# A new beginning and another order of block stages in a four-engine pipeline of two gated layers

## The chip, the cores and the metric

The program runs on one core of a Trainium2 chip. TensorE (PE) multiplies matrices into PSUM; VectorE (DVE), ScalarE (ACT) and GpSimd (POOL) work element by element, POOL on SBUF alone; SyncE (SP) issues most transfers. The metric is the device time of one execution in microseconds.

## The reference

```python
def _attn_ref(x, weight):                 # x: (2, 4096, 192), weight: (8, 7)
    w = weight - np.max(weight, axis=-1, keepdims=True)
    w = np.exp(w)
    w = w / (np.sum(w, axis=-1, keepdims=True) + 1e-09)
    x_pad = np.concatenate([np.zeros((B, pad, D), dtype=np.float32), x], axis=1)
    idx = np.arange(S)[:, None] + np.arange(K)[None, :]
    x_unf = x_pad[:, idx, :].reshape(B, S, K, H, group)
    out = np.einsum('hk,bskhg->bshg', w, x_unf)

def _moe_ref(x, w_in, w_out):             # x: (8192, 192), w_in: (192, 2048)
    h = x @ w_in
    relu6 = np.clip(h + 3.0, 0.0, 6.0)
    g = h * relu6 / 6.0
    return (g @ w_out).astype(np.float32)

def _moe2_ref(x, w_in, w_out, a, b):
    h = x @ w_in
    h2 = h * h
    h3 = h2 * h
    P = a[0] + a[1] * h + a[2] * h2 + a[3] * h3
    Q = 1.0 + np.abs(b[0]) * np.abs(h) + np.abs(b[1]) * h2
    g = P / (Q + 1e-06)
    return (g @ w_out).astype(np.float32)
```

The first function's result goes through the second and then the third: a causal convolution of 7 taps with softmax weights per head, then two layers 192 to 2048 to 192 with different gates.

## The kernel before

Channels lie on partitions: 128 upper ones ("a") and 64 lower ones ("b"). The 8192 positions are 16 blocks of 512 columns, two batches taking turns (`k.off % 2`). The 2048 hidden channels are 16 tiles of 128 (`NF`), so a block is 16 tiles and the whole 256 (`NT`). Every fp32 operand of a matmul is split in a rounded part (`_hi`) and a rest (`_lo`); `in_product` has five matmuls of 128x512 for a tile (hi x hi, lo x hi, hi x lo for the upper channels, two for the lower ones, whose hi and lo share one operand `xb_hl`), and `out_product` five into two accumulators, `y0a_acc` and `y0b_acc` for layer 1, `y1a_acc` and `y1b_acc` for layer 2. With four banks for `h`, that is all of PSUM.

A tile of layer 1 goes: `in1` (PE), `relu1` (ACT), `gate1` (DVE, in place in `r1`), `g1hi` (ACT), `g1lo` (POOL), `out1` (PE). A tile of layer 2: `in2`; `lin2`, `abs2`, `sq2` (ACT); `num2`, `num1` (DVE); `den_sum` (POOL); `rsq2`, `rec2` (ACT); `newton`, `g_first`, `g_neg` (DVE); `g2hi` (ACT), `g2lo` (POOL), `out2`.

The order of each engine's work is written out by hand in `SCHEDULE`: for each engine a list of stages with a lag, and `emit` goes through it once per step p, issuing each stage for tile p - lag. Layer 2's tiles come 21 steps after layer 1's. Block stages (the convolution's taps, roundings of a block's input, moving an accumulator out) stand in the same lists, with the steps of a block at which they come, and a parity where every second block is meant. `conv_b` treats the lower channels of two blocks at once, its taps 1 to 3 (`conv_b_head`) in steps 11 to 13, 4 to 6 (`conv_b_tail`) in 26 to 28 of 32. 64 steps are unrolled, then a loop of 32 steps runs, then the rest is unrolled; behind tile 255 the lists are sorted by `LATE`.

Weights arrive in 16 chunks (8 for each layer, two tiles of `w_in` and `w_out` in each) through three staging tiles. Chunk c is split at `weight_step(c)`: POOL rounds `win_hi`, ACT rounds `wout`, DVE computes `win_lo` and both `wout` rests (`w_lo`), and `w_done` lets PE use the chunk. Chunk 0 is split by POOL and ACT ahead of the steps. The prelude loads the taps, normalises them on DVE and ACT, computes the first block's convolution with upper and lower taps taking turns, and a few scalars of layer 2 (`root`).

## Time and profile before

| | us |
|---|---|
| median of 3 runs | 1306.22 |
| lowest, highest | 1304.28, 1306.86 |
| the profiled execution | 1306.78 |
| its span, first to last instruction | 1305.0 |

A row of the timeline gives start, duration, engine, line of the kernel, operation, what it writes and reads, the shape and, in brackets, how long its engine was idle before it and what ended that. DVE and ACT instructions overlap their neighbours a little, so that the distance from start to start is about 0.1 us less than the duration. A busy engine is therefore judged by those distances.

### The profile page before, as it was taken

Reading aid. Unit: us, or ns where it says so; the run is one execution under the profiler, and the core shown is the slowest. Engines: PE = TensorE matmul, PEld = TensorE weight load, DVE = VectorE, ACT = ScalarE, POOL = GpSimd, SP = SyncE. Lnnn points to the kernel's source line nnn. Section 1 sums busy time; section 2 is a strip of 40 time slices with the busy share of each in tenths; the row PEclk is TensorE's granted clock in tenths of the full one; section 3 lists DMA queues with packets and bytes.
Section 4 is the critical chain, followed back from the end, with each engine's and each line's share of the span. In section 5 each row is a group of like instructions: output and inputs, shape, how many; then the busy total and the mean of one; then the engine's idle time right before and its main releaser. Section 6 shows DMA issues by size and latency. Waiting matters only on the chain.

```text
span 1305.0 us, 19385 instructions
## 1 busy us (share of the span) xinstructions
PE 1211.6 (93%) x5120; PEld 960.1 (74%) x5120; DVE 1209.7 (93%) x1806; ACT 1174.2 (90%) x2207; POOL 1052.3 (81%) x822
## 2 busy tenths in 40 slices
PE   3788999999999999999999999999999999999776
PEld 2666777777778777777777777787777877888654
DVE  6789999999999999999999989999999999998787
ACT  3459999999999999999999999999999999999896
POOL 2567888888888888887898888888888888988665
PEclk9989999999999999999999999999999999999888
DMA  3230000010000000000000100000000000000000
GB/s 103 71 101 5 5 21 1 1 30 1 21 1 21 10 1 20 1 20 10 21 0 1 29 1 21 1 14 16 1 20 1 20 1 6 8 1 13 1 13 12
DMA packets 10005, 21.00 MB, mean 16 GB/s; under 512 B 1712, under 2 KB 1712, under 8 KB 9904
## 3 DMA queue, kind: packets, MB, share of 16 engines
q1 hardware_dynamic: 9904, 20.01, 5.4%
q14 instruction: 81, 0.66, 0.2%
q8 instruction: 20, 0.33, 0.1%
HBM read 13.72 MB, written 6.29 MB: 15 GB/s over the span
## 4 chain that ended last, share of the span: by engine, by line
DVE 41%; issue 24%; ACT 22%; PE 10%; POOL 1%; ACTq 1%; DVEq 0%; DMA 0%; SPq 0%; POOLq 0%
DVE num L336 8%; DVE h L368 6%; DVE g L375 5%; PE h L231 5%; ACT g_hi L392 5%; DVE conv_a L479 4%; ACT num L319 4%; DVE num L341 4%; DVE r L302 4%; ACT h L358 3%; DVE conv_b L490 3%; ACT sqr L330 3%; DVE den L363 3%; ACT r L296 2%; ACT rsq L352 2%
## 5 line engine op out<-in xcount | busy, mean ns | idle before, releaser
L348 POOL TENSOR_TENSOR den<-den,sqr 128x512 f32<-128x512 f32 x256 | 338.6, 1323 | 188.5 <-ACT sqr L330 166.5
L312 POOL TENSOR_TENSOR g_lo<-r,g_hi 128x512 fp32r<-128x512 f32 x256 | 345.9, 1351 | 34.1 <-ACT g_hi L392 33.4
L386 POOL TENSOR_TENSOR g_lo<-g,g_hi 128x512 fp32r<-128x512 f32 x256 | 332.0, 1297 | 2.5 <-ACT g_hi L392 2.5
L302 DVE SCALAR_TENSOR_TENSOR r<-r,h 128x512 f32<-128x512 f32 x256 | 174.9, 683 | 36.7 <-ACT r L296 36.6
L341 DVE SCALAR_TENSOR_TENSOR num<-num,coef,h 128x512 f32<-128x512 f32 x256 | 191.2, 747 | 8.6
L392 ACT ACTIVATE g_hi<-r 128x512 fp32r<-128x512 f32 x256 | 166.6, 651 | 29.5 <-DVE r L302 23.8
L368 DVE SCALAR_TENSOR_TENSOR h<-num,coef,h 128x512 f32<-128x512 f32 x256 | 191.4, 748 | 0.0
L336 DVE TENSOR_TENSOR num<-num,h 128x512 f32<-128x512 f32 x256 | 174.6, 682 | 16.0 <-issue 6.0
L358 ACT ACTIVATE h<-rsq 128x512 f32<-128x512 f32 x256 | 155.1, 606 | 37.7 <-DVE num L341 37.0
L363 DVE SCALAR_TENSOR_TENSOR den<-den,h 128x512 f32<-128x512 f32 x256 | 174.0, 679 | 10.4 <-ACT h L358 8.3
L319 ACT ACTIVATE num<-h,coef 128x512 f32<-128x512 f32 x256 | 179.6, 702 | 0.0
L352 ACT ACTIVATE rsq<-den 128x512 f32<-128x512 f32 x256 | 163.8, 640 | 16.5 <-POOL den L348 13.2
L375 DVE SCALAR_TENSOR_TENSOR g<-den,h 128x512 f32<-128x512 f32 x256 | 174.1, 680 | 0.5
L392 ACT ACTIVATE g_hi<-g 128x512 fp32r<-128x512 f32 x256 | 166.1, 649 | 3.5 <-PE y1b_acc L249 2.3
L325 ACT ACTIVATE den<-h 128x512 f32<-128x512 f32 x256 | 154.1, 602 | 11.5 <-DVE g L375 8.8
L296 ACT ACTIVATE r<-h 128x512 f32<-128x512 f32 x256 | 153.5, 600 | 7.4 <-PE h L231 7.2
L330 ACT ACTIVATE sqr<-h 128x512 f32<-128x512 f32 x256 | 154.2, 602 | 3.4 <-PE h L231 3.4
L231 PE MATMUL h<-x0a_hi,win_hi 128*128 128x512 f32 x256 | 109.1, 426 | 48.8 <-POOL wout L402 21.3
L231 PE MATMUL h<-x1a_hi,win_hi 128*128 128x512 f32 x256 | 102.2, 399 | 18.3 <-DVE g L375 17.0
L231 PEld LDWEIGHTS h<-x0a_hi,win_hi 128*128 128x128 f32 x256 | 48.4, 189 | 89.3 <-DVE r L302 45.9
L243 PE MATMUL y0a_acc<-g_hi,wout 128*128 128x512 f32 x256 | 101.8, 398 | 10.8 <-ACT y_a L408 8.1
L243 PE MATMUL y1a_acc<-g_hi,wout 128*128 128x512 f32 x256 | 101.7, 397 | 5.6 <-POOL g_lo L386 3.4
(88 smaller groups left out, 2925.9 us busy)
## 6 DMA issues: line engine op xcount, KB each, us to landing
stage_w<-w_pack SPq DMA_DIRECT2D x16, 448.0 KB, 3.3
raw_a<-x_a SPq DMA_DIRECT2D x16, 259.0 KB, 3.6
out<-y_a SPq DMA_DIRECT2D x16, 256.0 KB, 2.6
raw_b<-x_b SPq DMA_DIRECT2D x16, 129.5 KB, 2.8
out<-y_b SPq DMA_DIRECT2D x16, 128.0 KB, 2.4
coef<-coefs SPq DMA_DIRECT2D x1, 3.0 KB, 1.6
tap_a<-taps SPq DMA_DIRECT2D x1, 3.5 KB, 1.6
tap_b<-taps SPq DMA_DIRECT2D x1, 3.5 KB, 1.9
```

The source lines that it names most:

```text
L231: mm = eng.matmul(psum, w, x[:, :], start=(i == 0), stop=(i == len(passes) - 1))
L302: eng.scalar_tensor_tensor(out=r[:, :], in0=r[:, :], scalar=1.0, in1=h1_of(q), op0=ALU.min, op1=ALU.mult).then_inc(S["gate1"], 1)
L312: eng.tensor_tensor(g1_lo[q.off % 2][:, :], r1[q.off % 2][:, :], f32(g1_hi[q.off % 2][:, :]), ALU.subtract).then_inc(S["g1lo"], 1)
L319: eng.activation(num[q.off % 2][:, :], h2_of(q), ACT.Identity, bias=a2, scale=reg_a3) \
L336: eng.tensor_tensor(n, n, h2_of(q), ALU.mult).then_inc(S["num2"], 1)
L341: eng.scalar_tensor_tensor(out=n, in0=n, scalar=a1, in1=h2_of(q), op0=ALU.add, op1=ALU.mult).then_inc(S["num1"], 1)
L348: eng.tensor_tensor(d, d, sqr[q.off % 2][:, :], ALU.add).then_inc(S["den_sum"], 1)
L363: eng.scalar_tensor_tensor(out=d, in0=d, scalar=Q_ONE, in1=h2_of(q), op0=ALU.add, op1=ALU.mult).then_inc(S["newton"], 1)
L368: eng.scalar_tensor_tensor(out=h2_of(q), in0=num[q.off % 2][:, :], scalar=a0, in1=h2_of(q), op0=ALU.add, op1=ALU.mult).then_inc(S["g_first ...
L375: eng.scalar_tensor_tensor(out=g2[q.off % 2][:, :], in0=den[q.off % 2][:, :], scalar=2.0, in1=h2_of(q), op0=ALU.subtract, op1=ALU.mult) \
L386: eng.tensor_tensor(g2_lo[q.off % 2][:, :], g2[q.off % 2][:, :], f32(g2_hi[q.off % 2][:, :]), ALU.subtract).then_inc(S["g2lo"], 1)
L392: return eng.activation(dst, src, ACT.Copy)
```

## The change

The prelude takes other ways. SP issues the upper taps and the upper channels first, then the lower ones, then the coefficients; chunk 0 is issued from ACT's queue. DVE normalises the upper taps and runs all seven upper taps, then `win_lo` of chunk 0 and `x0a_lo`, then the lower taps. PE begins with the three upper passes of tiles 0 to 3, and does the two lower ones for each of these tiles in its step.

In the first 22 tiles `gate1` writes its result into an accumulator of layer 2, which is not in use yet, and `g1lo` is computed by DVE. Weights are split by other engines: both roundings by ACT, all three differences by POOL, and chunks 1 to 15 are spread evenly over steps 0 to 20. `w_done` becomes two semaphores, one for each half of a chunk. In `SCHEDULE` block stages stand at other places of the same step, and `sq2` ahead of `abs2`.

```diff
@@ -21,23 +21,26 @@
+EARLY = 22
...
-    "scalar": [("cs_b_hi", AHEAD, 13, 0), ("x2a_hi", SUM1, 1), ("x2b_hi", SUM1, 0),
...
+    "scalar": [("x2b_hi", SUM1, 0), ("cs_b_hi", AHEAD, 13, 0), ("y2a_out", SUM2, 0),
...
-    "gpsimd": [("den_sum", 21), ("g1lo", 0), ("x2a_lo", SUM1, 0), ("g2lo", 23), ("cs_a_lo", AHEAD, 10)],
+    "gpsimd": [("den_sum", 21), ("cs_a_lo", AHEAD, 10), ("g1lo", 0), ("g2lo", 23), ("x2a_lo", SUM1, 0)],
...
         def pe_in1(eng, q):
-            first_block_weights(eng, 0, q)
+            split = ("cs_a_hi", "cs_a_lo", "cs_b_lo")
+            if q.loop is None and q.off < H_BANKS:
+
+                if q.off == 0:
+                    for tile in range(H_BANKS):
+                        first_block_weights(eng, 0, Step(tile), "w_in_done")
+                        in_product(eng, 0, Step(tile), h1_of(Step(tile)), split, range(3))
+                in_product(eng, 0, q, h1_of(q), split, range(3, 5)).then_inc(S["h1_done"], 1)
+                return
+            first_block_weights(eng, 0, q, "w_in_done")
...
         def pe_out2(eng, q):
+            first_block_weights(eng, 1, q, "w_out_done")
+            if q.loop is None and q.off == 0:
+                eng.wait_ge(S["g1lo"], EARLY)
...
+        def gated(q):
+
+            return [ya_acc[1], yb_acc[1]][q.off % 2] if is_early(q) else r1[q.off % 2]
...
         def relu1(eng, q):
             wait_count(eng, S["h1_done"], q, 1)
-            wait_count(eng, S["g1lo"], q, -1)
+            wait_count(eng, S["gate1" if is_early(q) else "g1lo"], q, -1)
...
         def gate1(eng, q):
             wait_count(eng, S["relu1"], q, 1)
-            r = r1[q.off % 2]
-            eng.scalar_tensor_tensor(out=r[:, :], in0=r[:, :], scalar=1.0, in1=h1_of(q),
-                                     op0=ALU.min, op1=ALU.mult).then_inc(S["gate1"], 1)
+            if is_early(q):
+                wait_count(eng, S["g1lo"], q, -1)
+            eng.scalar_tensor_tensor(out=gated(q)[:, :], in0=r1[q.off % 2][:, :], scalar=1.0,
+                                     in1=h1_of(q), op0=ALU.min, op1=ALU.mult).then_inc(S["gate1"], 1)
...
         def g1lo(eng, q):
+            if is_early(q) != (eng is nc.vector):
+                return
+            if not is_early(q):
+                wait_count(eng, S["g1lo"], q, 0)
             wait_count(eng, S["g1hi"], q, 1)
...
-        def w_lo(eng, c):
-            hi, lo, wo, raw_in, raw_out = w_views(c)
+            round_hi(eng, hi, raw_in).then_inc(S["wi_hi"], 1)
+            round_hi(eng, wo[:, :, 0:DA + DB], raw_out).then_inc(S["wo_hi"], 1)
+
+        def w_lo_in(eng, c):
...
         def weight_step(c):
 
 
-            return 2 * (c - 1) if c <= n_chunks else NF - 2 + c - n_chunks
+            return (c - 1) * (IN2 - 1) // (n_layers * n_chunks - 2)
...
-            run(eng, SCHEDULE["vector"], lambda c: w_lo(eng, c))
+            run(eng, SCHEDULE["vector"])
...
-            w_hi(eng, 0, "in")
-            w_lo(eng, 0)
-            w_hi(eng, 1, "in")
-            run(eng, SCHEDULE["gpsimd"], lambda c: w_hi(eng, c, "in"), early=1)
+            w_lo_out(eng, 0)
+            run(eng, SCHEDULE["gpsimd"], lambda c: (w_lo_in(eng, c), w_lo_out(eng, c)))
```

PE's first instructions, before and after; `x0a_hi` is the rounded upper input, `x0b_hl` the lower one. Before:

```order
L231 MATMUL h<-x0a_hi,win_hi 128x512
L231 MATMUL h<-x0a_hi,win_lo 128x512
L231 MATMUL h<-x0a_lo,win_hi 128x512
L231 MATMUL h<-x0b_hl,win_hi 128x512
L231 MATMUL h<-x0b_hl,win_lo 128x512
L231 MATMUL h<-x0a_hi,win_hi 128x512
```

After, the upper passes of tile 3 and what follows them:

```order
L236 MATMUL h<-x0a_hi,win_hi 128x512
L236 MATMUL h<-x0a_hi,win_lo 128x512
L236 MATMUL h<-x0a_lo,win_hi 128x512
L236 MATMUL h<-x0b_hl,win_hi 128x512
L236 MATMUL h<-x0b_hl,win_lo 128x512
L236 MATMUL h<-x0b_hl,win_hi 128x512
```

The lower passes of a tile no longer follow its upper ones: twelve upper passes stand ahead of the first lower one.

DVE in the first steps, behind the prelude: `r` is what `gate1` writes. Before:

```order
L302 SCALAR_TENSOR_TENSOR r_0<-r_0,h 128x512
L400 SCALAR_TENSOR_TENSOR win_lo<-stage_w,win_hi 128x512
L400 SCALAR_TENSOR_TENSOR wout<-stage_w,wout 128x2x128
L400 SCALAR_TENSOR_TENSOR wout<-stage_w,wout 128x2x64
L302 SCALAR_TENSOR_TENSOR r_1<-r_1,h 128x512
L479 SCALAR_TENSOR_TENSOR conv_a<-raw_a,tap_a,conv_a 128x512
```

After:

```order
L327 SCALAR_TENSOR_TENSOR y1a_acc<-r_0,h 128x512
L341 TENSOR_TENSOR g_lo<-y1a_acc,g_hi 128x512
L327 SCALAR_TENSOR_TENSOR y1b_acc<-r_1,h 128x512
L508 SCALAR_TENSOR_TENSOR conv_a<-raw_a,tap_a,conv_a 128x512
L341 TENSOR_TENSOR g_lo<-y1b_acc,g_hi 128x512
```

The three weight differences between two gates are gone from DVE, and a `g_lo` stands behind each gate.

DVE at a step with one of the lower taps 1 to 3, from `g_neg` on (`g`), then the gate (`r`), `newton` (`den`), `g_first` (`h`). Before:

```order
L375 SCALAR_TENSOR_TENSOR g_0<-den,h 128x512
L302 SCALAR_TENSOR_TENSOR r_1<-r_1,h 128x512
L363 SCALAR_TENSOR_TENSOR den<-den,h 128x512
L368 SCALAR_TENSOR_TENSOR h<-num,coef,h 128x512
L490 SCALAR_TENSOR_TENSOR conv_b<-raw_b,tap_b,conv_b 128x512
```

After:

```order
L404 SCALAR_TENSOR_TENSOR g_0<-den,h 128x512
L327 SCALAR_TENSOR_TENSOR r_1<-r_1,h 128x512
L392 SCALAR_TENSOR_TENSOR den<-den,h 128x512
L519 SCALAR_TENSOR_TENSOR conv_b<-raw_b,tap_b,conv_b 128x512
L397 SCALAR_TENSOR_TENSOR h<-num,coef,h 128x512
```

The tap has moved ahead of `g_first`.

## Rows read from the trace of the kernel before

**Rows 1.** The page, section 1: busy us, share of the span, instructions.
```profile
PE 1211.6 (93%) x5120; PEld 960.1 (74%) x5120; DVE 1209.7 (93%) x1806; ACT 1174.2 (90%) x2207; POOL 1052.3 (81%) x822
```

**Rows 2.** Timeline, steps 5 and 6: start, us, engine, line, operation, [idle before].
```profile
40.82 0.51 ACT L392 ACTIVATE wout<-stage_w 128x384 fp32r<-128x384 f32 x1
41.24 0.58 ACT L296 ACTIVATE r<-h 128x512 f32<-128x512 f32 x1
...
41.85 0.69 DVE L302 SCALAR_TENSOR_TENSOR r<-r,h 128x512 f32<-128x512 f32 x1 [0.94 <-ACT r L296]
...
42.57 0.64 ACT L392 ACTIVATE g_hi<-r 128x512 fp32r<-128x512 f32 x1 [0.75 <-DVE r L302]
42.81 0.39 PE L231 MATMUL h<-x0b_hl,win_hi 128*128 128x512 f32 x1
...
43.34 1.78 DVE L400 SCALAR_TENSOR_TENSOR win_lo<-stage_w,win_hi 128x512 fp32r<-128x512 f32 x1
...
44.17 0.39 PE L249 MATMUL y0b_acc<-g_lo,wout 128*128 128x512 f32 x1
...
45.71 0.50 PE L231 MATMUL h<-x0a_hi,win_hi 128*128 128x512 f32 x1 [1.16 <-DVE wout L400]
```

**Rows 3.** Timeline, the prelude and the first tile.
```profile
2.13 0.43 SPq L565 DMA_DIRECT2D raw_a<-x_a  x1
...
6.12 0.49 DVE L497 TENSOR_SCALAR conv_a<-raw_a,tap_a 128x512 f32<-128x512 f32 x1 [0.63 <-DMA raw_a<-x_a]
...
11.00 1.75 DVE L490 SCALAR_TENSOR_TENSOR conv_b<-raw_b,tap_b,conv_b 128x512 f32<-128x512 f32 x1
...
21.29 0.79 PE L231 MATMUL h<-x0a_hi,win_hi 128*128 128x512 f32 x1 [21.29 <-POOL wout L402]
...
23.82 0.60 ACT L296 ACTIVATE r<-h 128x512 f32<-128x512 f32 x1 [4.29 <-PE h L231]
```

**Rows 4.** Timeline, out1 of the second block, and relu1 of tile 21.
```profile
78.79 0.77 PE L243 MATMUL y0a_acc<-g_hi,wout 128*128 128x512 f32 x1 [3.15 <-ACT y_a L408]
...
91.41 0.60 ACT L296 ACTIVATE r<-h 128x512 f32<-128x512 f32 x1 [0.43 <-PE h L231]
```

**Rows 5.** Busy time by stretch: stretch, us, then each engine, PEclk, DMA, GB/s.
```profile
23.80:91.40 67.60, 53.46 (x201) 40.18 (x201) 54.04 (x76) 34.95 (x64) 38.32 (x36) 0.95 0.29 90
...
296.60:1138.00 841.40, 818.80 (x3517) 652.49 (x3516) 802.96 (x1197) 795.16 (x1502) 714.66 (x551) 1.00 0.04 10
```

**Rows 6.** Groups of DVE instructions, 120 to 1200 us: busy us, mean ns, idle before.
```profile
L341 DVE SCALAR_TENSOR_TENSOR num<-num,coef,h 128x512 f32<-128x512 f32 x227 | 169.5, 747 | 7.5
...
L302 DVE SCALAR_TENSOR_TENSOR r<-r,h 128x512 f32<-128x512 f32 x227 | 155.1, 683 | 21.0 <-ACT r L296 21.0
...
L479 DVE SCALAR_TENSOR_TENSOR conv_a<-raw_a,tap_a,conv_a 128x512 f32<-128x512 f32 x78 | 72.2, 926 | 0.0
L490 DVE SCALAR_TENSOR_TENSOR conv_b<-raw_b,tap_b,conv_b 128x512 f32<-128x512 f32 x38 | 45.6, 1200 | 0.0
```

**Rows 7.** Timeline of DVE and of POOL, a step with a lower tap.
```profile
667.99 0.68 DVE L302 SCALAR_TENSOR_TENSOR r<-r,h 128x512 f32<-128x512 f32 x1
...
669.85 1.41 DVE L490 SCALAR_TENSOR_TENSOR conv_b<-raw_b,tap_b,conv_b 128x512 f32<-128x512 f32 x1
...
669.40 1.30 POOL L348 TENSOR_TENSOR den<-den,sqr 128x512 f32<-128x512 f32 x1 [0.90 <-ACT sqr L330]
```

**Rows 8.** Timeline, DVE and ACT in steps 21 and 22.
```profile
96.10 1.71 DVE L400 SCALAR_TENSOR_TENSOR wout<-stage_w,wout 128x256 fp32r<-128x256 f32 x2
...
99.29 0.60 ACT L358 ACTIVATE h<-rsq 128x512 f32<-128x512 f32 x1 [2.12 <-DVE num L341]
```

**Rows 9.** Timeline of DVE, the gate of step 3 of an odd block.
```profile
620.39 0.69 DVE L302 SCALAR_TENSOR_TENSOR r<-r,h 128x512 f32<-128x512 f32 x1 [1.29 <-ACT r L296]
```

**Rows 10.** Timeline of ACT and of DVE, rec2 and the gate of a step with a tap.
```profile
629.09 0.60 ACT L358 ACTIVATE h<-rsq 128x512 f32<-128x512 f32 x1 [0.42 <-DVE num L341]
...
629.51 0.68 DVE L302 SCALAR_TENSOR_TENSOR r<-r,h 128x512 f32<-128x512 f32 x1
```

108 lines of the change are left out of this document (61 added, 47 removed).

## Prediction

> **What bounds the kernel now.** I read the page first, for the shares of the engines, then the busy time by stretch, then the timeline of the beginning, and last two blocks of the middle instruction by instruction. A "step" is one round of the order table; relu1 of its tile marks it, and a block is 16 steps. PE and DVE are both at 93%, ACT at 90% [rows 1]: no engine alone is the bound. PE's work can't be shortened: from 42.81 to 44.17 the trace has six matmul starts' distances, 0.227 us each [rows 2], and 5120 of them are 1161 us. The rest of the 1305 is lost at four places. Nothing runs on PE before 21.29 [rows 3]. Then relu1 of tile 0 starts at 23.82 and that of tile 21 at 91.41 [rows 3, 4]: 21 steps in 67.6 us, 3.2 each, although layer 1 alone asks PE for 10 matmuls, 2.27 us; only 201 matmuls start there [rows 5]. In the middle 11 blocks take 841.4 us [rows 5] where 3520 matmuls need 798: 43 us lost, 3.9 for each block of 76.5. The fourth is the drain of layer 2 behind the last tile, whose order this change leaves alone.
>
> **The change, part by part.** The sum is made against the profiled execution, 1306.8 us (span 1305.0 and 1.8 around it); it stands 0.6 above the median of the runs, 1306.2.
>
> *The time to the first gate.* Before, the first tap starts at 6.12, when raw_a is there, 3.99 after its issue at 2.13 [rows 3], and the seven taps of the upper channels alternate with seven of the lower. Now raw_a is issued second and not fourth, about 0.9 earlier, so it is there at 5.2. Seven taps alone are 0.49 + 6 x 0.75 [rows 3, 6], each behind the one before it; a handover from one instruction to the next takes 0.03 [rows 2]: 5.2 us. POOL takes differences of chunk 0 meanwhile; what that does shows at 11.00, a tap of 1.75 beside POOL's win_lo [rows 3]. I add one such collision, 1.0. conv_a is ready at 11.4, its rounding (0.63, as g1hi [rows 2]) at 12.1, and PE starts its upper passes there instead of at 21.29. That head start is worth little by itself, since no gate can run before the lower passes: cs_a_lo 0.7, the second taps' three small operations 0.6 (an estimate, below the 0.49 of a 512-column one each), conv_b 5.2 with 1.5 for POOL's chunk 1, its two halves 0.63 and 0.7: 21.4. Two lower matmuls, 0.79 at the most each and overlapped [rows 3], put relu1 of tile 0 at 22.5 instead of 23.82: **1.3 us**, between 3.8 with no collision and a loss of 1 with twice as many.
>
> *Steps 0 to 20.* What spoils them is DVE. The gate waits behind win_lo, which took 1.78 because POOL computed g1lo at that time, and behind two wout differences; PE then waited 1.16 for w_done [rows 2]. The change takes these three from DVE and gives them to POOL, which loses g1lo for 22 tiles; DVE gets that. It reads one operand from PSUM, as gate1 does, whose mean is 683 ns over 227 tiles with POOL busy beside it [rows 6]: so early g1lo costs DVE 0.7 and should not collide. 0.6 + 0.7 and at most one tap are 2.1 us in a step.
>
> What is late next is ACT. Its chain in a step: relu1 starts, 0.61 later the gate, 0.72 later g1hi [rows 2], and 0.52 later ACT is free (a rounding's 0.63 less the overlap): 1.85. win_hi and wout_hi of a chunk now both stand behind g1hi, 0.52 + 0.42 from start to start [rows 2]; a step with a chunk is 2.8, one without is PE's 2.27. Chunks 2 to 15 lie in steps 0 to 19 at even distances: 14 x 2.8 + 7 x 2.27 = 55.1. At step 18 out1 waits for y1a_out; before, that was 3.15 of PE [rows 4], ACT being late; I take 1.5, since ACT stays nearly as loaded. POOL needs 1.3 for win_lo [rows 7] and, by columns, 1.0 for wout: 2.3 for a chunk, less than 2.8. 1 us for the taps that meet it. Together 57.6 instead of 67.6: **10.0 us**. If ACT's chunks fell wholly in its idle time it were 50.6 (17 gained); if each of 14 chunks exposed another 0.5, 64.6 (3 gained).
>
> *The weights' transfers.* Chunk 3's load now stands behind the second raw_b, which waits for the last conv_b tap, at about 20. With raw_a's 3.99 it is there at 24; ACT wants it in step 1, about 26, PE in step 6. Hidden; if it took twice as long, ACT would wait 2 us once, and PE would not.
>
> *Steps 21 to 23.* DVE still has wout differences of 1.71 in front of num here, and ACT waits 2.12 for num1 [rows 8]. They are gone. I take **2.5 us**, between 1 and 3.5, the latter with the win_lo ahead of them.
>
> *The middle.* Per step, nothing is added or removed; block stages change place.
> - Lower taps 1 to 3 (conv_b_head) stood behind g_first, when POOL is in den_sum: one took 1.41 at 669.85, den_sum having started at 669.40 [rows 7]. Now they stand between newton and g_first, 1.2 behind the start of the gate. In that step the gate starts at 667.99, POOL falls idle at 668.50 and den_sum starts at 669.40 [rows 7]: the tap's new place, 669.19, lies in POOL's gap. It begins first, and POOL is pushed back by 0.5, of which it has 0.9. Three taps save some 1.9 us of DVE (3 x (1.41 - 0.75) and less), of which PE gets 1.0.
> - In step 3 of an odd block both x2a_hi and cs_b_hi stood ahead of relu1, and DVE idled 1.29 before the gate [rows 9]. cs_b_hi comes behind relu1 now: 0.2 to 0.5.
> - y2b_sum stands no longer ahead of num1, cs_a_lo no longer behind g2lo but ahead of g1lo, whose reader has two steps: 0 to 0.3 together, or a loss of 0.2.
> - The taps of conv_a move by 0.6 from one side of newton to the other, within the same gap: nothing.
> Sum 1.4 us for a pair of blocks, which loses 8. Seven pairs lie between tile 21 and the drain: **10 us**. The most would be all collisions of taps, whose means are 926 and 1200 ns against 747 for the same instruction on PSUM [rows 6]: 78 x 0.18 + 38 x 0.45 = 31 us. In an order laid around gaps of tenths a loss of 10 is the other bound.
>
> The Trainium skill ("SBUF — State Buffer", section "Who interferes with whom") says that a DVE instruction with two SBUF inputs and a GpSimd instruction that reads SBUF exclude each other for the length of an instruction, and whichever starts first goes first; one with at most one SBUF input does not contend. The trace agrees: 1.75 and 1.41 for taps, 683 ns for the gate. By that rule the new beginning has a danger of its own, and it is rival 4.
>
> **Sum.** 1.3 + 10.0 + 2.5 + 10 = 23.8; 1306.8 - 23.8 = 1283.0 for a profiled execution, 1282.4 on the median's footing.
>
> **The rivals.**
> 1. *Only the beginning gains.* For it: in the middle DVE is busy 803 and ACT 795 of 841 us [rows 5], so a gap closed at one place opens at the next. Against it: what a collision adds is work on DVE, not waiting, and it vanishes. Time 1306.2 - 13.8 = 1292.
> 2. *The middle gains more*, since taps of conv_a fall in POOL's gap too where they now don't: 20 to 30 there, 1262 to 1272.
> 3. *Slower: newton loses its cover.* Before, a tap of conv_a between gate1 and newton gave ACT 0.66 more to finish rec2. At 629.09 rec2 starts, released by num1, and ends at 629.69; the gate at 629.51 ends about 630.11 [rows 10]: 0.42 to spare without the tap. ACT now does cs_b_hi and conv_b_first ahead of rec2, and a den_sum pushed back makes rsq2 later. What rec2 then comes late by more than 0.42 is lost in each of the nine tap steps of a block, 126 in all. At 0.11 us each the beginning's 13.8 is eaten; at 0.25 it is 31 us, 1323. Against it: rec2 waited for num1, not for rsq2 [rows 10].
> 4. *POOL's 42 weight differences hold the taps.* Each can hold a tap of the early steps for its 1.3 us. There are 12 such taps; all held cost 15.6 instead of my 1, the beginning gives nothing, the middle as forecast: 1296. For it: POOL works 32 us of 55 there. Against it: in most steps DVE waits for ACT anyway, 0.7 us.
>
> **How the numbers follow.** Forecast 0.45; rival 1 0.18; rival 2 0.17; rival 3 0.10, most of it over 1309; rival 4 0.10. The range holds the forecast, rivals 1 and 4 and the nearer part of rival 2: 1267 to 1297. A measurement of this kernel can tell 0.2%, 2.6 us, from no change: faster than 1303.6 0.88, within 0.04, slower 0.08.
>
> **What would show it.** First matmul near 12, relu1 of tile 0 near 22.5 and of tile 21 near 80, with ACT rather than DVE filled in the chunk steps. In the middle a block near 75.8, mean of the lower taps under 1000 ns, and POOL's den_sum lengthened in their place. Wrong would be: relu1 of tile 21 later than 86, the taps as long as before, or idle time before newton that rec2 ends.

## The result and the profile after

The changed kernel takes 1261.53 us (median; 1260.44 to 1261.88), the kernel before 1306.39 (1304.28 to 1306.86) beside it. The ratio is 0.9653, with a 95% interval of 0.964 to 0.9665: 45 us faster, where 24 were forecast, and 5.5 us below the lower end of the range, 1267. In the profiled executions the span went from 1305.0 to 1258.6 us, 46.4 less.

The page of the changed kernel, section 1, answers to [rows 1]:

```profile
PE 1197.9 (95%) x5120; PEld 964.5 (77%) x5120; DVE 1170.4 (93%) x1784; ACT 1170.5 (93%) x2223; POOL 1080.1 (86%) x828
```

DVE is busy for 39 us less and POOL for 28 us more. Of the work itself DVE gave up the weight differences and took 22 early `g1lo`; the rest is taps that became shorter and, on POOL, `den_sum` that became longer.

The starts of `relu1` in the two traces share out the 46.4 us (tile 0 and 21 of before in [rows 3, 4], tile 240 as the end of a stretch in [rows 5]):

| stretch | before, us | after, us | gain | forecast |
|---|---|---|---|---|
| to tile 0 | 23.8 | 22.7 | 1.1 | 1.3 |
| tiles 0 to 21 | 67.6 | 57.8 | 9.8 | 10.0 |
| tiles 21 to 24 | 15.6 | 13.9 | 1.7 | 2.5 |
| tiles 24 to 32 | 37.2 | 35.7 | 1.5 | |
| tiles 32 to 240 | 993.8 | 962.8 | 31.0 | 10 |
| from tile 240 | 166.9 | 165.6 | 1.3 | |

The beginning, which is the first three rows, came out near what was worked out, 12.6 us against 13.8. The forecast's 10 us for the middle are those of seven pairs of blocks, most of them in the stretch from tile 32 to 240. Nearly all of the error is there.

**The beginning.** The timeline of the changed kernel, prelude and first tile (start, us, engine, line, operation, idle before):

```profile
6.10 0.48 DVE L526 TENSOR_SCALAR conv_a<-raw_a,tap_a 128x512 f32<-128x512 f32 x1
6.61 5.10 DVE L508 SCALAR_TENSOR_TENSOR conv_a<-raw_a,tap_a,conv_a 128x512 f32<-128x512 f32 x6
...
12.52 0.77 PE L236 MATMUL h<-x0a_hi,win_hi 128*128 128x512 f32 x1 [12.52 <-ACT x0a_hi L421]
...
21.45 0.80 PE L236 MATMUL h<-x0b_hl,win_hi 128*128 128x512 f32 x1 [4.05 <-DVE x0b_hl L429]
...
22.71 0.60 ACT L320 ACTIVATE r<-h 128x512 f32<-128x512 f32 x1 [2.03 <-PE h L236]
```

This answers to [rows 3]. PE begins 8.8 us earlier, then stands again until the lower channels are rounded, and the first `relu1` comes 1.1 us earlier. The six upper taps take 0.85 each. The first of the seven still starts at 6.10, as before (6.12), although its channels were asked for 0.9 us earlier: they landed 4.6 us after the issue at 1.20, and DVE's list has an operation on the lower taps ahead of it, which waits for their transfer until 6.02.

Two steps of the early stretch, answering to [rows 2]:

```profile
40.72 1.30 POOL L431 TENSOR_TENSOR win_lo<-stage_w,win_hi 128x512 fp32r<-128x512 f32 x1 [2.11 <-ACT win_hi L421]
40.96 0.59 ACT L320 ACTIVATE r<-h 128x512 f32<-128x512 f32 x1
41.58 0.70 DVE L327 SCALAR_TENSOR_TENSOR y1b_acc<-r,h 128x512 f32<-128x512 f32 x1 [0.72 <-ACT r L320]
41.98 1.61 POOL L431 TENSOR_TENSOR wout<-stage_w,wout 128x256 fp32r<-128x256 f32 x2
42.18 1.08 DVE L508 SCALAR_TENSOR_TENSOR conv_a<-raw_a,tap_a,conv_a 128x512 f32<-128x512 f32 x1
```

The gate writes into an accumulator (`y1b_acc`), DVE waits for ACT before it, and the tap that meets POOL's differences takes 1.08 instead of 0.75. The 8 upper taps of that stretch have a mean of 1068 ns: 2.6 us of collisions in all, on an engine that waits for ACT anyway.

`out1` of the second block waited 3.15 [rows 4] and still waits, now 3.43; `relu1` of tile 21 is 10.9 earlier:

```profile
70.70 0.47 PE L248 MATMUL y0a_acc<-g_hi,wout 128*128 128x512 f32 x1 [3.43 <-ACT y_a L437]
...
80.53 0.60 ACT L320 ACTIVATE r<-h 128x512 f32<-128x512 f32 x1 [0.90 <-PE h L236]
```

**The middle.** Busy time by stretch (as [rows 5]; the second stretch is again 11 blocks):

```profile
22.70:80.50 57.80, 51.05 (x192) 37.78 (x192) 39.98 (x56) 40.68 (x78) 40.24 (x44) 0.91 0.35 113
277.20:1093.00 815.80, 807.87 (x3519) 656.38 (x3518) 784.89 (x1198) 786.99 (x1502) 739.52 (x551) 1.00 0.04 11
```

3520 matmuls at 0.227 us need 798 us, so 17.8 us are lost in 11 blocks where 43 were lost before. DVE has 18 us less to do for the same instructions, POOL 25 more. The groups of DVE, 120 to 1160 us, show whose they are:

```profile
L370 DVE SCALAR_TENSOR_TENSOR num<-num,coef,h 128x512 f32<-128x512 f32 x225 | 168.3, 748 | 8.0
...
L508 DVE SCALAR_TENSOR_TENSOR conv_a<-raw_a,tap_a,conv_a 128x512 f32<-128x512 f32 x78 | 58.3, 747 | 0.0
L519 DVE SCALAR_TENSOR_TENSOR conv_b<-raw_b,tap_b,conv_b 128x512 f32<-128x512 f32 x36 | 32.3, 898 | 0.0
```

Against [rows 6] the upper taps fell from 926 to 747 ns, which is what `num1` takes with an operand in PSUM, and the lower ones from 1200 to 898. The mean of 926 hides that only 31 of the 78 upper taps were long: all 26 of steps 1 and 4, at 1.23 to 1.28 us, and 5 of step 8 at 0.96. All 31 had started while POOL was in `g2lo`. The one of step 4, tile 68, before and then after:

```profile
317.29 1.31 POOL L386 TENSOR_TENSOR g_lo<-g,g_hi 128x512 fp32r<-128x512 f32 x1
317.91 1.25 DVE L479 SCALAR_TENSOR_TENSOR conv_a<-raw_a,tap_a,conv_a 128x512 f32<-128x512 f32 x1
```

```profile
298.52 0.75 DVE L508 SCALAR_TENSOR_TENSOR conv_a<-raw_a,tap_a,conv_a 128x512 f32<-128x512 f32 x1
298.86 1.57 POOL L377 TENSOR_TENSOR den<-den,sqr 128x512 f32<-128x512 f32 x1 [0.32 <-ACT den L354]
```

What was taken from the taps shows on POOL, whose `den_sum` is the page's first group, of before and then of after:

```profile
L348 POOL TENSOR_TENSOR den<-den,sqr 128x512 f32<-128x512 f32 x256 | 338.6, 1323 | 188.5 <-ACT sqr L330 166.5 <-ACT den L325 22.0
```

```profile
L377 POOL TENSOR_TENSOR den<-den,sqr 128x512 f32<-128x512 f32 x256 | 376.9, 1472 | 130.0 <-ACT den L354 129.1
```

And one place answers to [rows 7], a lower tap in its new place behind newton, with POOL beside it:

```profile
633.15 0.75 DVE L519 SCALAR_TENSOR_TENSOR conv_b<-raw_b,tap_b,conv_b 128x512 f32<-128x512 f32 x1
633.29 1.77 POOL L377 TENSOR_TENSOR den<-den,sqr 128x512 f32<-128x512 f32 x1 [0.22 <-ACT den L354]
```

The tap starts 0.14 ahead of `den_sum` and runs at its full speed; `den_sum` takes 1.77 instead of 1.30. Before, the tap started second and paid 1.41. POOL has idle time for it (130 us are left before `den_sum`), but it isn't free: ACT's `rsq2` waits 20.3 us for `den_sum` between 120 and 1160 us, where it waited 10.8.

Which waits this ended is in the views of waits (total, times, longest). ACT and DVE of the kernel before:

```profile
ACT h L358 <- DVE num L341: 37.0, 92, 2.1
```

```profile
DVE r L302 <- ACT r L296: 36.6, 50, 3.5
```

The same two of the changed kernel, and a third of its DVE:

```profile
ACT h L387 <- DVE num L370: 6.9, 21, 1.6
```

```profile
DVE den L392 <- ACT h L387: 13.7, 18, 2.8
...
DVE r L327 <- ACT r L320: 5.2, 18, 0.5
```

rec2 hardly waits for `num1` any more. The gate's wait for `relu1` fell too, but less than these two lines say, since the early gates stand under other names (`y1a_acc`, `y1b_acc`, 10.3 us together); between 120 and 1160 us it went from 20.5 to 4.6. Newton waits for rec2, 8.3 us in all before, and in those same limits nothing before and 6.7 now: rival 3's wait, though small. Where in a block the time went is best seen from the intervals between starts of `relu1`. This table is worked out from the traces: means over tiles 64 to 223, five pairs of blocks; the last row is a pair's length without rounding. An interval p goes from tile p of a block to the next. Intervals not listed differ by 0.1 or less.

| interval | before | after |
|---|---|---|
| 2 and 3, both blocks | 20.13 | 18.76 |
| 4 to 8 (upper taps 2 to 6), both | 47.35 | 46.28 |
| 10, first block | 5.11 | 5.15 |
| 11 to 14 (lower taps 1 to 3), first | 19.65 | 17.95 |
| 11 to 15, second | 24.40 | 23.87 |
| 0, first | 4.38 | 4.13 |
| a pair | 153.4 | 148.5 |

So a pair gains 5.0 us, where 1.4 were forecast. DVE's saving does not come back alike everywhere. The upper tap of step 4 is 0.5 us shorter in both blocks and that of step 8 on average 0.2 in the second, and intervals 4 to 8 are 1.1 shorter in all. That of step 1 is 0.49 shorter as well, and interval 1 stays at 5.65; with the taps alone moved (below) intervals 1 and 2 both stay as before, so nothing is gained there.

### The profile page after: what moved, and what is told of

Its sections match the earlier page's. It is cut to its first block, busy times and chain, and to the rows that moved or that the text cites. A ratio compares the mean times of both kernels' runs of the same rounds, so it can differ in the third digit from the quotient of the medians.

```text
span 1258.6 us, 19496 instructions
## 1 busy us (share of the span) xinstructions
PE 1197.9 (95%) x5120; PEld 964.5 (77%) x5120; DVE 1170.4 (93%) x1784; ACT 1170.5 (93%) x2223; POOL 1080.1 (86%) x828
## 4 chain that ended last, share of the span: by engine, by line
PE 49%; DVE 20%; ACT 14%; issue 13%; POOL 2%; ACTq 0%; DMA 0%; DVEq 0%; SPq 0%; POOLq 0%
PE h L236 25%; DVE num L365 4%; DVE g L404 4%; DVE h L397 3%; PE y0b_acc L253 3%; PE y0a_acc L248 3%; PE y0b_acc L254 3%; PE y0a_acc L250 3%; PE y0a_acc L249 2%; ACT g_hi L421 2%; PE y1a_acc L248 2%; ACT h L387 2%; ACT num L348 2%; PE y1a_acc L249 2%; PE y1a_acc L250 2%
## 5 line engine op out<-in xcount | busy, mean ns | idle before, releaser
L377 POOL TENSOR_TENSOR den<-den,sqr 128x512 f32<-128x512 f32 x256 | 376.9, 1472 | 130.0 <-ACT den L354 129.1
L415 POOL TENSOR_TENSOR g_lo<-g,g_hi 128x512 fp32r<-128x512 f32 x256 | 336.2, 1313 | 1.9 <-ACT g_hi L421 1.9
L341 POOL TENSOR_TENSOR g_lo<-r,g_hi 128x512 fp32r<-128x512 f32 x234 | 307.5, 1314 | 0.0
L327 DVE SCALAR_TENSOR_TENSOR r<-r,h 128x512 f32<-128x512 f32 x234 | 160.3, 685 | 6.9 <-ACT r L320 5.2
L421 ACT ACTIVATE g_hi<-r 128x512 fp32r<-128x512 f32 x234 | 154.8, 662 | 0.0
L236 PE MATMUL h<-x0a_hi,win_hi 128*128 128x512 f32 x256 | 103.7, 405 | 20.1 <-ACT x0a_hi L421 12.5
L236 PE MATMUL h<-x0b_hl,win_hi 128*128 128x512 f32 x256 | 101.4, 396 | 4.0 <-DVE x0b_hl L429 4.0
```

The lines of the kernel that those rows point to most:

```text
L236: mm = eng.matmul(psum, w, x[:, :], start=(i == 0), stop=(i == len(passes) - 1))
L341: eng.tensor_tensor(g1_lo[q.off % 2][:, :], gated(q)[:, :], f32(g1_hi[q.off % 2][:, :]), ALU.subtract).then_inc(S["g1lo"], 1)
L377: eng.tensor_tensor(d, d, sqr[q.off % 2][:, :], ALU.add).then_inc(S["den_sum"], 1)
L415: eng.tensor_tensor(g2_lo[q.off % 2][:, :], g2[q.off % 2][:, :], f32(g2_hi[q.off % 2][:, :]), ALU.subtract).then_inc(S["g2lo"], 1)
L421: return eng.activation(dst, src, ACT.Copy)
```

## The experiments

The kernel before, timed beside these runs, gave 1305.55 to 1306.1 us; differences written with + are against the changed kernel's 1261.53.

**The two halves.** First the new table alone in the kernel before:

```diff
-    "scalar": [("cs_b_hi", AHEAD, 13, 0), ("x2a_hi", SUM1, 1), ("x2b_hi", SUM1, 0),
+    "scalar": [("x2b_hi", SUM1, 0), ("cs_b_hi", AHEAD, 13, 0), ("y2a_out", SUM2, 0),
...
-    "vector": [("num2", 22), ("y2b_sum", SUM2, 0), ("cs_b_lo", AHEAD, 10, 1), ("num1", 22),
+    "vector": [("num2", 22), ("cs_b_lo", AHEAD, 14, 0), ("num1", 22),
...
-    "gpsimd": [("den_sum", 21), ("g1lo", 0), ("x2a_lo", SUM1, 0), ("g2lo", 23), ("cs_a_lo", AHEAD, 10)],
+    "gpsimd": [("den_sum", 21), ("cs_a_lo", AHEAD, 10), ("g1lo", 0), ("g2lo", 23), ("x2a_lo", SUM1, 0)],
```

> The kernel before with the changed SCHEDULE alone (old prelude, old split of the weights, g1lo on POOL throughout). The trace of after puts 31.0 us of the gain between relu1 of tile 32 and of tile 240, 14.0 ahead of tile 32 and 1.4 behind tile 240. If the two halves of the change are independent, this kernel keeps the 31: about 1275 us, ratio 0.976. If the middle only runs well because the new beginning leaves it in another phase, it stays above 1292.

Then the new beginning alone, which is the changed kernel with the same three lists turned back; its edit is the one above with - and + exchanged, `g1lo_early` kept.

> The changed kernel with the three old lists of SCHEDULE (g1lo_early kept, first in DVE's list). Independent halves: 14 us faster than before, about 1292 us, ratio 0.989, and the middle from tile 32 to tile 240 takes 994 us as before. If the halves need each other: over 1300.

Measured: the table alone 1273.49 us (ratio 0.9751 [0.9733, 0.9769]), 32.6 less; the beginning alone 1293.37 (0.9906 [0.989, 0.9923]), 12.7 less. The halves add up to 45.3, and the whole gave 44.9: no interaction shows. From tile 32 to 240 the table alone needs 962.1 us and the beginning alone 993.4, which are the changed kernel's 962.8 and the old kernel's 993.8. The middle's 31 us are the table's.

**One engine's list undone in the changed kernel.** First DVE's (`"vector"`), its first and last rows being:

```diff
-    "vector": [("g1lo_early", 1), ("num2", 22), ("cs_b_lo", AHEAD, 14, 0), ("num1", 22),
+    "vector": [("g1lo_early", 1), ("num2", 22), ("y2b_sum", SUM2, 0), ("cs_b_lo", AHEAD, 10, 1), ("num1", 22),
...
-               ("g_first", 22)],
+               ("cs_b_lo", AHEAD, 14, 0)],
```

> The changed kernel with DVE's list as before. Theory A (the middle's gain is DVE work that collisions with POOL no longer lengthen: tap means 926 to 754 and 1200 to 907 ns, together 24.5 us): this kernel loses 20 to 28 of the 31, 1282 to 1290 us, with the tap means back near 926 and 1200. Theory B (the gain is ACT's chain: cs_b_hi behind relu1, block stages in another order): it loses under 8, below 1270.

Then ACT's (`"scalar"`):

```diff
-    "scalar": [("x2b_hi", SUM1, 0), ("cs_b_hi", AHEAD, 13, 0), ("y2a_out", SUM2, 0),
+    "scalar": [("cs_b_hi", AHEAD, 13, 0), ("x2a_hi", SUM1, 1), ("x2b_hi", SUM1, 0),
...
-               ("conv_a_first", AHEAD, 1), ("sq2", 21), ("abs2", 21), ("cs_a_hi", AHEAD, 10),
+               ("rec2", 22), ("conv_b_first", PAIR_AHEAD, 11, 0), ("abs2", 21), ("sq2", 21),
```

> The changed kernel with ACT's list as before. Theory A (DVE and POOL collisions): loses 3 to 8 us, 1265 to 1270, taps stay short. Theory B (ACT's chain): loses 20 or more, above 1280, while the taps stay short.

Measured: DVE's list undone 1297.75 us (0.9937 [0.992, 0.9953]), +36; ACT's undone 1273.74 (0.9751 [0.9735, 0.9768]), +12. The first is more than the whole table is worth. The trace of that kernel says why: DVE's groups, 150 to 1100 us, and ACT's waits:

```profile
L508 DVE SCALAR_TENSOR_TENSOR conv_a<-raw_a,tap_a,conv_a 128x512 f32<-128x512 f32 x77 | 63.7, 827 | 5.3 <-ACT conv_a L525 5.3
L519 DVE SCALAR_TENSOR_TENSOR conv_b<-raw_b,tap_b,conv_b 128x512 f32<-128x512 f32 x36 | 46.7, 1297 | 0.0
```

```profile
ACT h L387 <- DVE num L370: 58.5, 125, 1.6
```

rec2's wait for `num1` is back, and the old DVE list with the new ACT list has a wait of its own, for the first upper tap (`conv_a_first`), which ACT now does behind rec2. A second such wait is that of `y2b_sum`, which stands early in the old DVE list, for ACT's `y2b_move`, which stands later in the new ACT list: 9.6 us in 13 blocks between 120 and 1160 us, against 2.8 before and 0.3 in the changed kernel. What a list costs when it is undone alone is thus not what it is worth: mismatches with the other list are in it. ACT's list undone cost more than the 0.2 to 0.5 per pair of the prediction, so one more cause had to be there.

**The taps, one group at a time.** Lower taps 1 to 3 (`conv_b_head`) back behind `g_first`; the upper taps back ahead of newton; the last lower taps (`conv_b_tail`) back behind the gate:

```diff
-               ("conv_b_head", PAIR_AHEAD, (11, 12, 13), 0), ("conv_b_tail", AHEAD, (10, 11, 12), 0),
-               ("g_first", 22)],
+               ("conv_b_tail", AHEAD, (10, 11, 12), 0),
+               ("g_first", 22), ("conv_b_head", PAIR_AHEAD, (11, 12, 13), 0)],
```

> The changed kernel with one move undone: lower taps 1 to 3 (conv_b_head) behind g_first again. Theory A (a tap that starts while POOL is in den_sum waits for it): those 19 taps grow from 750 to about 1400 ns, 12 us of DVE, and the kernel is 7 to 12 us slower, 1268 to 1274. Rival (PE and ACT have slack there, what counts is ACT's order): under 3 us slower, below 1264.5.

```diff
-               ("y2b_sum", SUM2, 0), ("gate1", 0), ("newton", 22), ("conv_a", AHEAD, (1, 4, 5, 6, 7, 8)),
+               ("y2b_sum", SUM2, 0), ("gate1", 0), ("conv_a", AHEAD, (1, 4, 5, 6, 7, 8)), ("newton", 22),
```

> The changed kernel with one move undone: the upper taps 1 to 6 between gate1 and newton again. As predicted on record, both places lie in POOL's gap and this changes nothing: 1261 to 1263. Theory A taken to all taps (conv_a's mean fell from 928 to 747 ns, 14 us of DVE in 77 taps, because this move took them out of POOL's g2lo): 8 to 14 us slower, 1269 to 1275.

```diff
-               ("y2b_sum", SUM2, 0), ("gate1", 0), ("newton", 22), ("conv_a", AHEAD, (1, 4, 5, 6, 7, 8)),
-               ("conv_b_head", PAIR_AHEAD, (11, 12, 13), 0), ("conv_b_tail", AHEAD, (10, 11, 12), 0),
-               ("g_first", 22)],
+               ("y2b_sum", SUM2, 0), ("gate1", 0), ("conv_b_tail", AHEAD, (10, 11, 12), 0),
+               ("newton", 22), ("conv_a", AHEAD, (1, 4, 5, 6, 7, 8)),
+               ("conv_b_head", PAIR_AHEAD, (11, 12, 13), 0), ("g_first", 22)],
```

> The changed kernel with one move undone: lower taps 4 to 6 (conv_b_tail) between gate1 and newton again. Theory A: these 18 taps meet g2lo in about half the cases (0.5 us each), 2 to 5 us slower, 1264 to 1266. Rival (their old place was free, as assumed in the prediction): 1261 to 1263.

Measured: 1272.56 (0.9747 [0.9729, 0.9766]), +11.0; 1269.96 (0.9725 [0.9707, 0.9743]), +8.4; 1265.12 (0.969 [0.9671, 0.971]), +3.6. Head and tail came as the first theory said. In the run with the head back its taps take 1202 ns on average with the tail's, as before, and intervals 11 to 14 of the first block make 19.7 instead of 17.95: 1.8 us of PE's time for 1.8 of DVE's (the three taps take 4.14 instead of 2.31). The upper taps are the forecast's "nothing", and 8.4 us fall to them; in their trace:

```profile
L508 DVE SCALAR_TENSOR_TENSOR conv_a<-raw_a,tap_a,conv_a 128x512 f32<-128x512 f32 x77 | 63.6, 826 | 5.3 <-ACT conv_a L525 5.3
```

79 ns longer each over 77 taps are 6.1 us, all of it in the taps of step 4 (1.18 and 1.27 us); those of step 1 take 0.75 here, since they first wait for `conv_a_first`, which makes the 5.3 us. Intervals 4 to 8 grow from 46.3 to 47.1 per pair, and the two intervals numbered 2 by 0.7; that part belongs to the wait, not to the collision. So of the 8.4 us some five are the collision's, and the rest is the new ACT list's.

The three groups together, added to the kernel before, with nothing else moved:

```diff
-               ("conv_b_tail", AHEAD, (10, 11, 12), 0), ("conv_a", AHEAD, (1, 4, 5, 6, 7, 8)),
-               ("newton", 22), ("g_first", 22), ("conv_b_head", PAIR_AHEAD, (11, 12, 13), 0),
+               ("newton", 22), ("conv_a", AHEAD, (1, 4, 5, 6, 7, 8)),
+               ("conv_b_head", PAIR_AHEAD, (11, 12, 13), 0), ("conv_b_tail", AHEAD, (10, 11, 12), 0), ("g_first", 22),
```

> The kernel before with only the three groups of taps (conv_a, conv_b_head, conv_b_tail) moved on DVE to their place between newton and g_first. The three moves undone one by one in the changed kernel cost 11, 8 and 4 us. Theory A (collisions, each with its own price): this kernel is 17 to 25 us faster than before, 1281 to 1289, tap means near 750 and 900 ns. Rival (the moves need ACT's and POOL's new lists to pay, since the new places make newton wait for rec2 or den_sum late for rsq2): under 10 us, above 1296.

1289.26 (0.9873 [0.9857, 0.989]), 16.8 less, just short of the 17 expected. The upper taps have 745 ns there, the lower ones 1054, where 900 was expected: tap 1 starts while POOL is in `cs_a_lo` and takes 1.67; with the whole table it takes 0.81. Intervals 4 to 8 give the same 1.0 per pair as the whole change, and 11 to 14 of the first block 1.3 instead of 1.7. So the taps are worth about 17 of the table's 32.6, and 16 were still to be found.

**The square ahead of the absolute value.** ACT's `abs2` writes `den`, whose last reader is DVE's gate of layer 2 (`g`) a step earlier; `sq2` waits for nothing of DVE. The prediction has no term for this swap. Undone in the changed kernel, and beside it `cs_b_hi` put back ahead of `relu1`, the only move of ACT's that the prediction had priced:

```diff
-  ("conv_a_first", AHEAD, 1), ("sq2", 21), ("abs2", 21), ("cs_a_hi", AHEAD, 10),
+  ("conv_a_first", AHEAD, 1), ("abs2", 21), ("sq2", 21), ("cs_a_hi", AHEAD, 10),
```

> The changed kernel with one pair put back on ACT: abs2 ahead of sq2 in each step. Theory S (what is new since the prediction): abs2 writes the tile of den whose last reader is DVE's gate of the step before, so ACT stood 0.6 to 0.8 us at step 2 of each block until DVE had written g; with sq2 ahead, the square fills that time, since it waits for nothing DVE makes. Put back, steps 2 to 3 lengthen by 0.6 to 0.75 us and each of some 14 blocks costs that: 1268 to 1272 us. Rival T: the gap is bridged anyway because DVE, with faster taps, finishes its gate sooner: under 2 us, 1261 to 1263.5. The step periods at 2 and 3 tell them apart.

```diff
-  ("rsq2", 22), ("relu1", 0), ("conv_b_first", PAIR_AHEAD, 11, 0), ("cs_b_hi", AHEAD, 3, 1), ("rec2", 22),
+  ("cs_b_hi", AHEAD, 3, 1), ("rsq2", 22), ("relu1", 0), ("conv_b_first", PAIR_AHEAD, 11, 0), ("rec2", 22),
```

> The changed kernel with one step put back on ACT: the upper half of x0b (cs_b_hi of step 3, every second block) ahead of rsq2 and relu1. The prediction gave 0.2 to 0.5 us per pair of blocks. By that, some 7 pairs, 1262.5 to 1265 us. Rival: ACT has the time at that step, no change, 1261 to 1262. If theory S (the square ahead of the absolute value) carries only half of what the ACT list cost (12.2 us), this must give 5 or more: 1266 to 1268.

Measured: 1270.27 (0.9729 [0.9713, 0.9745]), +8.7, which carries most of the ACT list's 12.2; and 1261.01 (0.9663 [0.9646, 0.968]), no change. The step of tile 66 with `abs2` first, and then the same step of the changed kernel:

```profile
289.15 0.69 DVE L404 SCALAR_TENSOR_TENSOR g<-den,h 128x512 f32<-128x512 f32 x1
...
289.94 0.60 ACT L354 ACTIVATE den<-h 128x512 f32<-128x512 f32 x1 [0.32 <-DVE g L404]
```

```profile
287.68 0.69 DVE L404 SCALAR_TENSOR_TENSOR g<-den,h 128x512 f32<-128x512 f32 x1
...
288.00 0.64 ACT L359 ACTIVATE sqr<-h 128x512 f32<-128x512 f32 x1
...
288.48 0.64 ACT L354 ACTIVATE den<-h 128x512 f32<-128x512 f32 x1
```

With `abs2` first ACT stands for 0.32 us until `g` is written. With `sq2` first the square runs under `g`, and the absolute value follows it without a gap. ACT's waits for `g` are 2.6 us in all in the changed kernel and 11.2 with `abs2` first. The intervals numbered 2 are 5.04 there against 4.61 in both blocks, 0.43 each (0.6 to 0.75 was expected), and interval 10 of the first block is 5.68 against 5.15, of which more below.

**Does the same move help the kernel before?** To the kernel before with its taps moved, first the swap was added:

```diff
-  ("conv_b_first", PAIR_AHEAD, 11, 0), ("abs2", 21), ("sq2", 21),
+  ("conv_b_first", PAIR_AHEAD, 11, 0), ("sq2", 21), ("abs2", 21),
```

> The kernel before with two moves: the three groups of taps on DVE (worth 16.8 us by themselves) and the square ahead of the absolute value on ACT. Theory S: the two add, 16.8 and 7 to 10, so 1279 to 1283 us. If the square's place matters only together with the other moves of the ACT list: 1287 to 1290, as with the taps alone.

Then `cs_b_hi` of step 3 as well:

```diff
-  ("cs_b_hi", AHEAD, 3, 1), ("y1a_out", SUM1, 0), ("y2b_move", SUM2, 0),
+  ("y1a_out", SUM1, 0), ("y2b_move", SUM2, 0),
...
-  ("rec2", 22), ("conv_b_first", PAIR_AHEAD, 11, 0),
+  ("cs_b_hi", AHEAD, 3, 1), ("rec2", 22), ("conv_b_first", PAIR_AHEAD, 11, 0),
```

> As the run before, and in addition the upper half of x0b behind relu1 and conv_b's first tap on ACT. The whole order table is worth 32.6 us. If three moves are all that matters of it: 1274 to 1277 us. If the rest (the sums of the second output's lower half, the accumulators moved out in another order, POOL's list) carries a share of its own: 1278 to 1283.

Measured: 1287.94 (0.9869 [0.9852, 0.9885]) and 1288.99 (0.9863 [0.9842, 0.9884]): 1.3 and 0.3 less than the taps alone, which is within the noise. The first run's theory S was missed, and its other branch had the time but not the cause, since the partner is a move of DVE's; of the second both branches were missed. The swap, worth 8.7 in the changed kernel, is worth 1 here. The intervals of the first of them say what happened. The two numbered 2 gain 0.5 and 0.4, as they should, and interval 10 of the first block grows from 5.11 to 5.73 on average: in four of seven pairs of blocks it is 6.2, in the others 5.03. From tile 32 to 240 the swap does gain 3.7 us (973.4 against 977.1), and 2.9 are lost behind tile 240, a stretch that takes 165 to 168 us in all these kernels without a pattern. In interval 10 the trace shows (first block, tile 74):

```profile
338.35 0.67 DVE L336 TENSOR_TENSOR num<-num,h 128x512 f32<-128x512 f32 x1
...
339.05 1.85 DVE L400 SCALAR_TENSOR_TENSOR x0b_hl<-conv_b,x0b_hl 64x512 fp32r<-64x512 f32 x1
...
340.94 0.75 DVE L341 SCALAR_TENSOR_TENSOR num<-num,coef,h 128x512 f32<-128x512 f32 x1
...
341.78 0.60 ACT L358 ACTIVATE h<-rsq 128x512 f32<-128x512 f32 x1 [1.44 <-DVE num L341]
```

`cs_b_lo`, the lower channels' remainder, has two inputs in SBUF, meets POOL's `g1lo`, takes 1.85 us, and stands ahead of `num1`, for which rec2 waits 1.44. With the taps alone it is the other way round, in the same place:

```profile
339.99 0.69 DVE L400 SCALAR_TENSOR_TENSOR x0b_hl<-conv_b,x0b_hl 64x512 fp32r<-64x512 f32 x1
...
340.05 1.78 POOL L312 TENSOR_TENSOR g_lo<-r,g_hi 128x512 fp32r<-128x512 f32 x1
```

There `cs_b_lo` starts 0.06 ahead of POOL and runs bare. With the swap the two start together, and in the four pairs with an interval of 6.2 it takes 1.85, in the other three 0.69. With `cs_b_hi` moved too it takes 1.85 in all seven. So what the swap changed is who begins first. The changed kernel's DVE list has `cs_b_lo` behind `num1`. That was another move that the prediction had not priced. It was added to the kernel before with taps and swap:

```diff
-  ("y2b_sum", SUM2, 0), ("cs_b_lo", AHEAD, 10, 1), ("num1", 22), ("x2b_res", SUM1, 0), ("x2b_lo", SUM1, 0),
+  ("y2b_sum", SUM2, 0), ("num1", 22), ("x2b_res", SUM1, 0), ("cs_b_lo", AHEAD, 10, 1), ("x2b_lo", SUM1, 0),
```

> The kernel before with three moves: the taps on DVE, the square ahead of the absolute value on ACT (as in the run at 1287.9 us), and on DVE conv_b's lower remainder of step 10 (cs_b_lo) behind num1 instead of ahead of it. In the run without this third move ACT's reciprocal (rec2) at step 10 of every second block stood 0.9 to 1.4 us for DVE's num1, and the interval to the next gate grew from 5.11 to 6.21 us, which took back what the square's place gave at step 2. Theory L: those two moves belong together; the interval goes to 5.1 to 5.7 us and the time to 1280 to 1284 us. Rival: POOL's list (cs_a_lo late) keeps it at 6.2 us, 1287 to 1289 us.

And it was undone in the changed kernel:

```diff
-  ("num1", 22), ("x2b_res", SUM1, 0), ("cs_b_lo", AHEAD, 10, 1), ("x2b_lo", SUM1, 0),
+  ("cs_b_lo", AHEAD, 10, 1), ("num1", 22), ("x2b_res", SUM1, 0), ("x2b_lo", SUM1, 0),
```

> The changed kernel with that one move undone: conv_b's lower remainder of step 10 ahead of num1 on DVE. Theory L: rec2 waits for num1 at step 10, one interval of each pair of blocks grows by 0.5 to 1.1 us, so 7 or 8 times that: 1265 to 1270 us. Rival: num1 has the time, no change, 1261 to 1262.5 us.

Measured: 1282.11 (0.9815 [0.9799, 0.9832]), 5.8 less than without it; interval 10 falls back to 5.15. And 1264.15 (0.9679 [0.9662, 0.9695]), +2.6, a little under the expected 1265: interval 10 grows to 6.18, but in the two pairs from tile 32 to 95 it stays at 5.03, and there `cs_b_lo` took 0.69 instead of 1.84. Swap and `cs_b_lo` together bring 7.1 us to the kernel that had only the taps, while the swap alone brought 1.3. `cs_b_lo` alone was not run on that kernel; but interval 10, which hardly varies within most of the kernels, tells the two moves apart:

| interval 10, first block | `cs_b_lo` ahead of `num1` | behind `num1` |
|---|---|---|
| `abs2` first | 5.11 (before, and taps alone) | 5.68 (swap undone, and ACT's list undone) |
| `sq2` first | 5.03 or 6.2 | 5.15 (changed kernel, and three moves) |

Behind `num1` it starts 0.7 to 0.8 us into POOL's `g1lo`, takes 1.06 to 1.15 and makes `g` late instead. With `abs2` first ACT then waits 0.96 for `g`, with `sq2` first 0.37. Tile 74 of the changed kernel with the swap undone:

```profile
325.96 1.13 DVE L429 SCALAR_TENSOR_TENSOR x0b_hl<-conv_b,x0b_hl 64x512 fp32r<-64x512 f32 x1
...
327.91 0.60 ACT L354 ACTIVATE den<-h 128x512 f32<-128x512 f32 x1 [0.96 <-DVE g L404]
```

Either move alone can lengthen this interval by about half a microsecond or more; the two together don't.

**The beginning, in parts.** The early gates undone (with chunk 1 split ahead of the loop), and PE's first four tiles in whole products instead of all upper passes first:

```diff
-EARLY = 22
+EARLY = 0
...
+            w_lo_in(eng, 1)
+            w_lo_out(eng, 1)
...
```

> The changed kernel with g1lo of all tiles on POOL (EARLY = 0, chunk 1 split on POOL ahead of the steps, nothing else). If the early gates in the accumulators carry the beginning: POOL then needs 1.3 + 2.3 us in a chunk step, 3.6 instead of ACT's 2.8, so relu1 of tile 21 comes 8 to 15 us later and the kernel ends at 1269 to 1276. If ACT's chain of 2.8 binds anyway: under 3 us slower.

```diff
-            if q.loop is None and q.off < H_BANKS:
+            if False:
```

> The changed kernel in which PE does each of the first four tiles whole, as before (no twelve upper passes ahead of the lower ones). The lower input is the last to arrive, so only the three upper passes of tile 0 come behind it, and three more for each of tiles 1 to 3 at the slow cadence of 0.43: relu1 of tile 0 is 1.3 us later, that of tile 3 up to 4; since ACT's 2.8 per step binds, 1 to 3 us slower in all, 1262.5 to 1264.5. If the idle PE also loses its clock: more than 4.

Measured: 1274.37 (0.9757 [0.9741, 0.9773]), +12.8; and 1260.77 (0.9653 [0.9637, 0.9669]), no change, where 1 to 3 us were expected. Without early gates tiles 0 to 21 take 67.3 us, as in the kernel before (67.6): PE waits for POOL's `g_lo`, all but once before tile 21,

```profile
PE y0a_acc L248 <- POOL g_lo L341: 13.5, 13, 1.9
```

since POOL has both the weight differences and `g1lo` and is busy for 63.2 of the 67.3 us. The new split of the weights with `g1lo` left on POOL is thus worth nothing in that stretch; only with `g1lo` on DVE does it pay. Whether `g1lo` on DVE would pay with the old split was not run. PE's early upper passes are worth nothing either, since PE is not what is late in these steps: tiles 0 to 21 take 57.7 us without them and 57.8 with them.

**Two tries to go below the changed kernel.** A wait of PE left in the middle was `out1`'s for `y1a_out`, 3.4 us in four places, 0.9 at most; the expectation below counts it in each block, which is more than the trace shows. ACT's two stages (and in the second kernel DVE's two as well) were put a step earlier:

```diff
-    "scalar": [("x2b_hi", SUM1, 0), ("cs_b_hi", AHEAD, 13, 0), ("y2a_out", SUM2, 0),
-               ("y1a_out", SUM1, 0), ("x2a_hi", SUM1, 1), ("y2b_move", SUM2, 0), ("rsq2", 22),
+    "scalar": [("cs_b_hi", AHEAD, 13, 0), ("y2a_out", SUM2, 0),
+               ("x2a_hi", SUM1, 1), ("y2b_move", SUM2, 0), ("rsq2", 22),
...
-               ("lin2", 21), ("g1hi", 0), ("g2hi", 23)],
+               ("lin2", 21), ("x2b_hi", SUM1 - 1, 0), ("y1a_out", SUM1 - 1, 0), ("g1hi", 0), ("g2hi", 23)],
```

> The changed kernel with layer 1's accumulators moved out one step earlier on ACT: x2b_hi and y1a_out behind lin2 of step 17 instead of at the head of step 18. PE waits for y1a_out 1.04 us in each block (0.88 of idle and a restart). If ACT's program order is what delays it, this wait goes: 8 to 15 us faster than the changed kernel, 1247 to 1254. If ACT's 1 us more ahead of g1hi and g2hi only moves the wait to g1lo and g2lo, it stays within 3 us.

In the second kernel DVE's list, in addition (and on ACT `x2b_hi` ahead of `cs_a_hi`):

```diff
-    "vector": [("g1lo_early", 1), ("num2", 22), ("cs_b_lo", AHEAD, 14, 0), ("num1", 22),
-               ("x2b_res", SUM1, 0), ("cs_b_lo", AHEAD, 10, 1), ("x2b_lo", SUM1, 0), ("g_neg", 23),
+    "vector": [("g1lo_early", 1), ("num2", 22), ("x2b_lo", SUM1, 0), ("cs_b_lo", AHEAD, 14, 0), ("num1", 22),
+               ("cs_b_lo", AHEAD, 10, 1), ("g_neg", 23),
...
-               ("g_first", 22)],
+               ("g_first", 22), ("x2b_res", SUM1 - 1, 0)],
```

> The run before last moved x2b_hi and y1a_out one step earlier on ACT, and PE's wait of 0.88 us for y1a_out became one of 1.06 for x1b_hl, which DVE writes. Here DVE's x2b_res and x2b_lo also come earlier (behind g_first of step 17, behind num2 of step 18). If DVE's place is all that held PE: 7 to 13 us faster than the changed kernel, 1249 to 1255. If the steps are full, so that the wait appears at another stage again: within 3 us.

Measured: 1260.50 (0.9653 [0.9634, 0.9673]) and 1263.02 (0.9666 [0.965, 0.9682]), no gain. In the first the wait only changed its name:

```profile
PE y0b_acc L253 <- DVE x1b_hl L463: 7.0, 8, 1.6
```

PE now waits for the lower accumulator instead of the upper one. None of the kernels that were run beats the changed kernel measurably.

## Why the prediction was wrong, step by step

- **First gate, 1.3 us.** 1.1 measured; first matmul 12.5 (12.1 forecast), tile 0 at 22.7 (22.5). One term failed: the first tap was to start at 5.2 and started at 6.10, behind the wait for the lower taps' transfer. The upper taps and their collision with POOL then took 5.6 us for 6.2, and the rest 0.4 less than its sum. That start scatters between kernels with the same prelude (21.7 to 22.7 in the runs), so the closeness is luck.
- **Steps 0 to 20, 10.0 us.** 9.8 measured, 57.8 us for 57.6. ACT's chain set the pace as said: a step with a chunk took mostly 2.8. Two terms were off and cancelled: `out1`'s wait in the second block was taken at 1.5 and was 3.43, while five steps without a chunk took 1.85, ACT's chain alone, and not PE's 2.27. The early gates' share was seen rightly, since the run without them lost all of it.
- **Steps 21 to 23, 2.5 us.** 1.7 measured, and 2.1 with the beginning alone (15.6, 13.9 and 13.5 us), within the bounds of 1 to 3.5. The weights' transfers stayed hidden: no wait for one stands in the trace behind the prelude's taps.
- **The middle, 10 us.** 31 measured. Four steps of it failed:
  - *"The taps of conv_a move by 0.6 ... within the same gap: nothing."* The old place was not in POOL's gap: the taps of steps 1 and 4 started while POOL was in `g2lo`, 31 of 78 were long, and 926 ns against 747 [rows 6] are 14 us of DVE. The new place removed all of it. PE got about half: 1.1 us per pair, some 7 in all, from the taps of steps 4 and 8, and nothing from those of step 1. Put back, the taps cost 8.4 us, a part of which is a wait that the new ACT list adds.
  - *conv_b_head, "1.9 us of DVE, of which PE gets 1.0".* DVE saved 1.7 per pair, and intervals 11 to 14 are 1.7 shorter; undone it is 1.8 for 1.8. The halving had no row behind it. In these steps rec2 waited for `num1` (21.3 us in all with the head back, 6.9 in the changed kernel), newton follows rec2 and `g` follows newton, so that DVE's taps lay on the chain that sets the step.
  - *`sq2` ahead of `abs2`* stands in the account of the change, and had no term. It is worth 8.7 us in the changed kernel. Its wait was in the trace of before: ACT waited 8.8 us for `g` there, 14 times.
  - *`cs_b_hi`, 0.2 to 0.5 a pair*, was priced and is worth nothing measurable, while `cs_b_lo` behind `num1` was not priced and gave 2.6 us in one kernel and 5.8 in the other.

  That the middle came out at the 31 us which the prediction gave as "the most" is chance: that sum was of collisions alone, and the taps by themselves gave 16.8.
- **The rivals.** Rival 2 was the nearest to what happened: the upper taps did fall into a better place, and the middle gave 31 where it said 20 to 30. It had 0.17, and the range cut through it. The upper taps are only some 7 of it, though, and the swap stood in no rival. Rival 1 fell: what was gained at one place was not lost at the next. Rival 3's wait appeared (DVE's newton on rec2, 6.7 us in the middle, from nothing) but at no size that outweighed the gains. Rival 4 fell: early upper taps took 1068 ns, 0.32 over their bare time, 2.6 us in all and 0.7 more for the three lower ones, instead of 15.6. Its rule as the prediction quoted it, from the Trainium skill ("SBUF — State Buffer", section "Who interferes with whom"), held: the early `g1lo` with one operand in PSUM took 684 to 687 ns beside a busy POOL, and which of tap and `den_sum` started first decided who paid (0.75 and 1.77, against 1.41 and 1.30 before). Both delays are 0.1 to 0.2 us short of a full wait for the other's end.

**What stays open.** The taps, the swap and `cs_b_lo` together give some 23.5 of the table's 32.6 us (1282.1 against 1273.5). The other 8.6 lie with the moves that were not tried apart: `cs_b_lo` of step 14, `y2b_sum`, the order in which ACT empties the accumulators, `conv_b_first` and `conv_a_first` on the two sides of rec2, and POOL's list. From tile 32 to 240 the two kernels differ by 8.1 us, mostly in interval 11 of the first block (5.23 against 4.87), 2 and 3 of the second (9.38 against 9.07), and 0 of the first (4.30 against 4.11). Nor is it shown why the 0.49 us that the tap of step 1 lost brought PE nothing.

## What to carry to other kernels

Where an instruction's mean stands above that of the same instruction with an operand elsewhere, look step by step for the ones that are long, and see what the other engine does when they start. Count their difference as gain to be had, and ask for each step whether the engine sets the pace there; let the chance of it follow from where the new place lies against the other engine's start, not from how far the code moved. List every move of a reordered table, give each a term, and look for the wait that it touches: two neighbours swapped on one engine were worth 8.7 us. And price moves in sets: the same swap was worth 1 us in one kernel and 9 in another, in part because on its own it turned round who began first elsewhere.

## What the runs showed of the hardware

- A DVE tap with both inputs in SBUF (128x512, 747 ns alone) took 1400 to 1590 ns where it started while POOL was in `den_sum` (12 taps of the kernel before), and 1250 to 1630 with the lower taps put back (18 taps); where the tap began first it took 750, and `den_sum` 1770 instead of 1300. The total is about the same (2.71 and 2.52 us); the place in the order decides which engine pays. A start together can fall either way: 0.69 or 1.85 us for the same `cs_b_lo` in one trace.
- PE's upper passes ahead of everything start 0.42 to 0.43 us apart from 13.09 to 16.50 and 0.23 to 0.28 behind that (0.227 in steady work [rows 2]), although the trace shows a granted clock of 1.00 throughout. Then PE is idle for 4.05 us. Behind this pause the trace shows 0.50, the 1.2 GHz level, and the matmuls start 0.43 apart until 30. In the kernel with whole products it shows 1.00 from 21 to 30, but there too the matmuls start 0.43 apart, from 21.4 to 26.1, and 0.23 only then. So in the first 26 us a clock of 1.00 in these views can't be taken for the full one; the starts tell. Busy time by stretch, changed kernel and then the one with whole products (12 matmuls in 5 us, then 19 in 4):

```profile
12.50:16.40 3.90, 3.88 (x9) 3.08 (x10) 3.72 (x7) 2.39 (x5) 2.56 (x3) 1.00 0.00 0
...
21.40:26.00 4.60, 3.39 (x7) 2.31 (x8) 2.46 (x8) 2.53 (x6) 0.73 (x1) 0.50 0.79 255
26.00:30.00 4.00, 4.00 (x11) 2.93 (x11) 2.95 (x4) 3.08 (x7) 4.00 (x6) 0.50 0.20 50
```

```profile
21.00:26.00 5.00, 5.00 (x12) 3.93 (x13) 2.81 (x8) 3.16 (x6) 1.37 (x2) 1.00 0.72 230
26.00:30.00 4.00, 4.00 (x19) 3.23 (x19) 2.83 (x5) 3.08 (x7) 3.85 (x5) 1.00 0.34 106
```

  With the early passes the slow starts thus last some 4 us longer. It costs nothing here: tiles 0 to 4 take 10.46 us with them and 10.45 without, since ACT's chain sets these steps.
- One POOL instruction of 128x512 took 1.29 to 1.31 us where DVE took 0.68 for the same difference (`g1lo`) with one operand in PSUM. So the stage took half the time on DVE, which waited for ACT in these 22 tiles.
